# Scatter behind the first level, folds dealt evenly, and experts walked in their own order

## The reference

```python
# 1. delta-rule attention; B, H, S, D = 4, 8, 768, 48
k_n = k / (norm(k) + 1e-6)
for t in range(S):
    y[t] = q[t] @ state
    state = state + beta[t] * outer(k_n[t], v[t] - k_n[t] @ state)
x = y as (3072 tokens, 384)
# 2. dense part, d_model 384, d_ff 1024
h = (x @ w1) * (x @ w2) @ w3
x = h @ w_out
# 3. 8 experts, one for each token
logits = x @ w_gate + modality_bias[modality_id]
e_idx = argmax(logits);  gate_w = softmax(logits)[e_idx]
out[token] = gate_w * (relu(x @ moe2_w1[e_idx]) @ moe2_w2[e_idx])
```

## Time and profile before

| what | value |
|---|---|
| runs | 986.44, 989.28, 988.99 us; median 988.99 us |
| profiled execution | 982.71 us, its span 980.8 us |
| PE busy | 889.7 us (91%) |
| DVE, ACT, POOL busy | 497.3, 343.7, 277.7 us |
| DMA | 60.13 MB, mean 61 GB/s |
| mean granted clock of TensorE | 0.955 |
| last dense product ends, about | 678 us |
| first down products of the expert stage | 727.4 us |

### The profile page before, as it was taken

The page is one execution under the profiler, slowest core; times in us unless marked ns, Lnnn a source line. Parts: engine busy times, 40 slices in busy tenths (PEclk is TensorE's granted clock), DMA queues, the critical chain, the costliest instruction groups (busy, mean ns, idle before and its releaser), DMA issues.

```text
span 980.8 us, 29550 instructions
## 1 busy us (share of the span) xinstructions
PE 889.7 (91%) x11972; PEld 746.7 (76%) x11973; DVE 497.3 (51%) x891; ACT 343.7 (35%) x628; POOL 277.7 (28%) x296
## 2 busy tenths in 40 slices
PE   4898878999998999899989999997369999999996
PEld 3666556778876887688768878986259898989985
DVE  2456656665675567556755673232356333333332
ACT  1234343443554355435533442221153222222221
POOL 5333333444434443444344421010001101011010
PEclk9999986999999999999989999998579999999998
DMA  7333211111111111111111101100941111111110
GB/s 248 104 103 113 75 37 37 38 38 38 47 39 58 38 44 42 59 38 46 40 59 30 29 23 46 32 34 18 320 181 44 42 42 41 38 41 41 48 42 21
DMA packets 46570, 60.13 MB, mean 61 GB/s; under 512 B 9192, under 2 KB 39160, under 8 KB 45552
## 3 DMA queue, kind: packets, MB, share of 16 engines
q1 hardware_dynamic: 38640, 42.35, 14.4%
q0 software_dynamic: 3200, 9.56, 2.6%
q10 hardware_dynamic: 4608, 6.46, 2.5%
HBM read 42.26 MB, written 11.77 MB: 55 GB/s over the span
## 4 chain that ended last, share of the span: by engine, by line
PE 76%; POOL 7%; DVE 6%; issue 5%; ACT 3%; DMA 1%; SPq 1%; ACTq 0%; POOLq 0%; DVEq 0%
PE banks L1418 17%; PE banks L1543 12%; PE banks L1557 11%; PE banks L1436 10%; PE banks L1278 4%; PE banks L1388 3%; PE banks L1355 2%; PE banks L1574 2%; PE banks L1345 2%; PE banks L1367 2%; PE banks L1238 2%; POOL nm L535 1%; POOL inv L539 1%; DVE corr L873 1%; POOL sorted_rows L555 1%
## 5 line engine op out<-in xcount | busy, mean ns | idle before, releaser
L1418 PE MATMUL banks<-xr,w12r 128*128 128x512 f32 x864 | 226.4, 410 | 0.0
L1418 PEld LDWEIGHTS banks<-xr,w12r 128*128 128x128 f32 x864 | 159.9, 193 | 35.9 <-DVE xr L933 0.2
L1543 PE MATMUL banks<-experts,kept 128*128 x486 | 124.6, 411 | 11.0 <-DVE experts L1170 8.5
L1543 PEld LDWEIGHTS banks<-experts,kept 128*128 128x128 f32 x486 | 92.6, 195 | 32.3 <-issue 11.6
L1557 PE MATMUL banks<-experts,kept 128*128 x624 | 114.8, 340 | 0.0
L1436 PE MATMUL banks<-kept,hr 128*128 128x392 f32 x576 | 112.2, 347 | 0.0
L1557 PEld LDWEIGHTS banks<-experts,kept 128*128 128x128 f32 x624 | 107.1, 188 | 0.0
L1436 PEld LDWEIGHTS banks<-kept,hr 128*128 128x128 f32 x576 | 100.9, 188 | 2.0
L585 POOL DMA_INDIRECT out<-ys,xs x26 | 25.6, 984 | 259.8 <-DVE ys L1205 259.8
L523 POOL TENSOR_TENSOR kb<-keys,beta_sb 128x384 f32<-128x384 f32 x24 | 29.1, 1214 | 245.5 <-PE banks L1377 245.5
L621 ACT ACTIVATE inv<-banks 128x512 f16<-128x512 f32 x96 | 57.2, 596 | 84.9 <-PE banks L1278 72.4
(11 more groups left out here) (144 smaller groups left out, 1338.9 us busy)
## 6 DMA issues: line engine op xcount, KB each, us to landing
raw<-in_moe_w SPq DMA_DIRECT2D x6, 1536.0 KB, 7.3
kq<-in_qT SPq DMA_DIRECT2D x24, 256.0 KB, 2.7
xs<-sorted_rows ACTq DMA_DIRECT2D x28, 197.0 KB, 2.4
kraw<-in_k SPq DMA_DIRECT2D x24, 192.0 KB, 2.3
vals<-in_v SPq DMA_DIRECT2D x48, 96.0 KB, 2.5
w3T<-in_w3T SPq DMA_DIRECT2D x8, 512.0 KB, 4.4
w<-in_w SPq DMA_DIRECT2D x8, 384.0 KB, 4.7
xT<-yT SPq DMA_DIRECT2D x48, 64.0 KB, 2.1
```

What stands on the lines that cost most here:

```text
L1418: last = mm(psum[:, UP + w, :], w12r[:, p, w, k, j * P:(j + 1) * P], xr[:, r, k, :], start=(k == 0 and p == r), stop=(k == KT - 1 and p == 1))
L1543: last = mm(psum[:, f, :], xsr[:, w, p, k, :], experts[:, bass.ds(slot * (2 * WE) + at, FF // 2)], start=(k == 0 and p == r), stop=(k == K ...
```

## The change

Four parts.

- **Scatter.** POOL's `scatter` of turn u moves to turn u+1, behind `first_level` and ahead of `square`.
- **Gates and folds.** The 24 gate products of turn 0 are dealt four to each of the six slots. The 64 fold products are dealt evenly over the 30 slots of turns 1 to 5. Copies and loads follow the block that ends.
- **Experts in their own order.** The table's expert is the expert's number; the tile count of an expert is at least one; SP loads experts 0 to 7 without conditions. Ten operations on VectorE that made ranks are gone.
- **Early loads and splits.** `xs` and `raw` change places in memory. SP loads experts 0 and 1 when attention has ended; ScalarE and VectorE split expert 0 at pieces 17, 20 and 21 of the last group; expert 1 is split by ScalarE behind the last `exps` (w1) and behind the first two tiles' rows (w2), by VectorE behind these rows (w1) and the first hidden values (w2). `table[3]` starts at 1, so tile 0 splits nothing.

```diff
@@ -35,6 +35,7 @@
 PIECES = 24
 FIRST_GROUP = 6
 FIRST_SLOT = 2
+FOLD_SLOTS = SPLITS * (FIRST_GROUP - 1)
 E_SCALE = 1024.0
 ROW = WX + 2
 GATE, TOKEN = WX, WX + 1
@@ -48,6 +49,7 @@
 NO_TOKEN = 1 << 20
 
 ROWS = (18, 19, 22, 23)
+FIRST_SPLITS = {17: ("w1", 0), 20: ("w1", 1), 21: ("w2", 0)}
 CHOOSE, EXPS, COUNT, WEIGH, RANK = 2, 3, 4, 6, 9
 
 
@@ -184,8 +186,8 @@
         late = ExitStack()
         experts = sbuf(late, "experts", [P, SLOTS * 2 * WE], F32R)
         hid = sbuf(late, "hid", [P, FF])
+        xs = sbuf(late, "xs", [P, TURN, ROW])
         raw = sbuf(late, "raw", [P, SLOTS * WE])
...
         def gates_of(u, at):
 
-            return range(8 * (at // 2), 8 * (at // 2) + 8) if u == 0 and at % 2 else range(0)
+            return range(4 * at, 4 * at + 4) if u == 0 else range(0)
 
         def folds_of(u, at):
 
-            half = (0, None, 1, 2, None, 3)[at] if at != 1 and at != 4 else None
-            if half is None or not 1 <= u <= 4:
-                return []
-            i = 2 * (u - 1) + half // 2
-            return [(i, half % 2)]
+            n = SPLITS * (u - 1) + at
+            return range(FT * FT * n // FOLD_SLOTS, FT * FT * (n + 1) // FOLD_SLOTS) if 0 <= n < FOLD_SLOTS else range(0)
+
+        def folds_ended(u, at):
+
+            return [n // FT for n in folds_of(u, at) if n % FT == FT - 1]
+
+        def fold_turn(i):
+
+            return next(u for u in range(1, FIRST_GROUP) for at in range(SPLITS) if i in folds_ended(u, at))
 
         def piece_of(u, at):
...
                     load_k(u + 3)
-                for n in (2 * u - 1, 2 * u):
-                    if W_SLOTS <= n < FT:
+                for n in range(W_SLOTS, FT):
+                    if u == fold_turn(n - W_SLOTS) + 1:
                         load_w3(n)
+                    if n in (2 * u - 1, 2 * u):
                         load_w12(n)
                 if live(u) and u:
                     load_v(u)
...
                 sp.wait_ge(sent[b], 64 * C)
             sp.wait_ge(q["y_taken"], UNITS + 1)
+            def load_expert(k):
+
+                for at, size, name in ((0, KT * FF, "w1"), (KT * FF, FT * DM, "w2")):
+                    since(sp, q[f"expert_{name}_in"], 16 * k)
+                    if k >= SLOTS:
+                        sp.wait_ge(q[f"lower_{name}"], (k - SLOTS + 1) * (2 if name == "w1" else 1))
+                    at_slot = k % SLOTS * WE + at
+                    sp.dma_start(raw[:, at_slot:at_slot + size], a[f"moe2_{name}"][k]
+                                 ).then_inc(q[f"expert_{name}_in"], 16)
+
             sp.dma_start(fill[:], a["fill"]).then_inc(q["b_in"], 16)
             sp.dma_start(numbers[:], a["small"][:, M_STARTS:]).then_inc(q["b_in"], 16)
 
 
+            for k in range(SLOTS):
+                load_expert(k)
             sp.wait_ge(q["b_in"], 80)
             sp.dma_start(sorted_rows[E * CAP:E * CAP + P, :], fill[:, :].bitcast(F32)
                          ).then_inc(q["filled"], 16)
 
             fill_after(sp, range(0, E, 2))
 
-            sp.wait_ge(q["ranks_ready"], 1)
-            for k in range(E):
-                e = sp.value_load(table[0:1, 2, k:k + 1], min_val=0, max_val=E - 1)
-                some = sp.value_load(table[0:1, 2, E + k:E + k + 1], min_val=0, max_val=1)
-                with sp.If(some > 0):
-                    at_slot = k % SLOTS * WE
-                    for at, size, name in ((0, KT * FF, "w1"), (KT * FF, FT * DM, "w2")):
-                        if k == 0 and name == "w2":
-
-                            for w in range(2):
-                                sp.wait_ge(x_in[w], 16)
-                        if k:
-
-                            sp.wait_ge(q[f"expert_{name}_in"], 16 * k)
-                        if k >= SLOTS:
-
-                            sp.wait_ge(q[f"lower_{name}"], (k - SLOTS + 1) * (2 if name == "w1" else 1))
-                        sp.dma_start(raw[:, at_slot + at:at_slot + at + size],
-                                     a[f"moe2_{name}"][bass.ds(e, 1)].rearrange("o p n -> p (o n)")
-                                     ).then_inc(q[f"expert_{name}_in"], 16)
+            for k in range(SLOTS, E):
+                load_expert(k)
 
 
         @block.gpsimd
...
             def turn(u):
                 if live(u):
                     first_level(u)
+                for at in range(SPLITS):
+                    piece = piece_of(u - 1, at)
+                    if piece and piece[0] and piece[1] == RANK:
+                        scatter(piece[0] - 1)
                 if live(u + 2):
                     square(u + 2)
                 if live(u + 1):
@@ -566,10 +582,6 @@
                     beta_keys(u + 1)
                 if live(u + 2):
                     normalise(u + 2)
-                for at in range(SPLITS):
-                    piece = piece_of(u, at)
-                    if piece and piece[0] and piece[1] == RANK:
-                        scatter(piece[0] - 1)
 
             nc.gpsimd.memset(keys[:, :, D:PAD], 0.0).then_inc(q["key_pad_clear"], 1)
...
                 for c in group_begun(u, at, 2):
                     split_x(c)
+
+            def upper_ahead(rank, name, f=0):
+                act.wait_ge(q["up_b"], FT * C)
+                if rank:
+                    act.wait_ge(q["down_done"], B * C)
+                act.wait_ge(q[f"expert_{name}_in"], 16 * (rank + 1))
+                src, upper, _ = ahead_of(rank, name, f)
+                nc.scalar.activation(upper, src, ACT.Copy).then_inc(q[f"upper_{name}"], 1)
 
             def turn(u):
                 if live(u - 1):
@@ -766,6 +787,8 @@
             for u in range(-2, last_turn() + 1):
                 turn(u)
             exps(C - 1)
+            upper_ahead(1, "w1", 0)
+            upper_ahead(1, "w1", 1)
 
 
...
@@ -800,13 +823,10 @@
             act.wait_ge(q["filled"], 16 * (E + 1))
             load_x(0, 0)
             load_x(1, 1)
-            first = act.value_load(table[0:1, 3, 0:1], min_val=0, max_val=E - 1)
-            split(first, "w1", [0])
             take_x(0, 0)
-            split(first, "w1", [1])
             take_x(1, 1)
+            upper_ahead(1, "w2")
             take_hid(0)
-            split(first, "w2")
 
...
@@ -1029,12 +1049,16 @@
 
                 v.tensor_copy(place[:], lred[:, 4]).then_inc(q["place_ready"], 1)
 
+            def lower_ahead(rank, name, f=0):
+                dve.wait_ge(q[f"upper_{name}"], 2 * rank + f + 1 if name == "w1" else rank + 1)
+                src, upper, lower = ahead_of(rank, name, f)
+                nc.vector.tensor_tensor(lower, src, upper, ALU.subtract).then_inc(q[f"lower_{name}"], 1)
+
...
@@ -1113,45 +1139,32 @@
             v.tensor_tensor(fill_at[:], small[:, M_PLACE:M_PLACE + E], total, ALU.add
                             ).then_inc(q["fill_ready"], 1)
             link(v.tensor_reduce(ntile[:, 0], over[:], AX.X, ALU.add))
-            link(v.tensor_scalar(ntile[:, 1], ntile[:, 0], 0.0, None, ALU.is_gt))
-
-            link(v.tensor_copy(ntile[:, 2:4, 0:1], ntile[:, 0:2, 0:1]))
+            link(v.tensor_scalar(ntile[:, 0], ntile[:, 0], 1.0, None, ALU.max))
+
+            link(v.tensor_copy(ntile[:, 1, 0:1], ntile[:, 0, 0:1]))
             for e in range(1, E):
-                link(v.tensor_tensor(ntile[:, 2:4, e:e + 1], ntile[:, 2:4, e - 1:e], ntile[:, 0:2, e:e + 1],
-                                     ALU.add))
+                link(v.tensor_tensor(ntile[:, 1, e:e + 1], ntile[:, 1, e - 1:e], ntile[:, 0, e:e + 1], ALU.add))
             tiles = numbers[:, M_TILE - M_STARTS:M_TILE - M_STARTS + TABLE * E].rearrange("p (i e) -> p i e", e=E)
 
-            def by_tile(k, n=TABLE):
-                return ntile[:, None, k, :].to_broadcast([P, n, E])
-
-
-            link(v.tensor_tensor(past[:, 0, 0:E], tiles[:, 0:E], by_tile(3, E), ALU.is_ge))
-            link(v.tensor_reduce(ttab[:, 0, 0:E], past[:, 0, 0:E], AX.X, ALU.add))
-            v.tensor_scalar(table[:, 2, 0:E], ttab[:, 0, 0:E], float(E - 1), None, ALU.min)
-            link(v.tensor_scalar(ttab[:, 2, 0:E], numbers[:, M_TILE - M_STARTS:M_TILE - M_STARTS + E * E:E],
-                                 ntile[:, 3, E - 1:E], None, ALU.is_lt))
-            v.tensor_copy(table[:, 2, E:2 * E], ttab[:, 2, 0:E]).then_inc(q["ranks_ready"], 1)
-            v.tensor_copy(table[:, 2, 2 * E:2 * E + 1], ntile[:, 2, E - 1:E])
-
-
-            link(v.tensor_tensor(past[:, 0], tiles, by_tile(2), ALU.is_ge))
+            def by_tile(k):
+                return ntile[:, None, k, :].to_broadcast([P, TABLE, E])
+
+            v.tensor_copy(table[:, 2, 2 * E:2 * E + 1], ntile[:, 1, E - 1:E])
+
+
+            link(v.tensor_tensor(past[:, 0], tiles, by_tile(1), ALU.is_ge))
             link(v.tensor_tensor(past[:, 1], past[:, 0], by_tile(0), ALU.mult))
             link(v.tensor_reduce(ttab[:, 0], past[:, 0], AX.X, ALU.add))
             link(v.tensor_reduce(ttab[:, 1], past[:, 1], AX.X, ALU.add))
```

(31 more changed lines are left out.)

29 lines of the change are left out of this document (19 added, 10 removed).

## The result

**Slower, as forecast, by a little more.** The changed kernel takes 1054.94 us (median of 4 runs, 1054.72 to 1055.84), the kernel before 987.72 (4 runs, 986.05 to 989.28): ratio 1.0683, 95% interval 1.0659 to 1.0706. Forecast were 1049 us and a range of 1028 to 1075. The profiled execution took 1054.83 us, its span is 1053.0 us. In the frame of profiled executions, where the sum was made, 1042.3 stood against 1054.8: the sum was 12.5 us short, and half of that was made up in the total by the 6.3 us added for the median. The kernel after doesn't show such a difference (its median and its profiled execution agree).

A forecast was written before the change was run, and what follows sets the result against it. TensorE bounds the expert stage, a chain of small products and copies the attention turns. 982.7 + 87 (stalled tiles) - 12.4 (early loads) - 15 (folds) + 0 (scatter) = 1042.3; plus 6.3 for the median: 1049 us, range 1028 to 1075.

The forecast's parts named there:

- 6.3 us added for the median: Whole kernel: the median of the runs lies 6.3 us above the profiled execution, taking 1042.3 to 1049.
- 31 tiles, 16 transfers, five stalls: Expert stage: five empty experts add tiles, 26 to 31; tiles with a split just begun stall, 87 us in all.
- 17.4 us a stalled tile: One-tile experts: split ready at +6.5, then 8.8, plus 2.1 for the clock; bounds 15.3 and 24.1.
- Rivals 1 (no stall): Expert stage: splits keep ahead, so extra tiles cost 48 us instead of 87; total 1010, chance 6%.
- 2 (low clock throughout, 24.1): Expert stage: TensorE at the low level all through one-tile experts, 34 us more; total 1082, chance 9%.
- rival 4: Expert stage: an empty expert takes no tile after all, leaving only -12.4 and -15; total 962, chance 3%.
- Smaller folds and gates, -15: Attention turns 0 to 6: evenly dealt products shorten gaps on the chain, -15 us; bounds -21 and -5.
- Rival 3: Attention turns 0 to 5: smaller folds give nothing because TensorE's waits keep the clock low; total 1064, chance 9%.
- Early loads and splits, -12.4: Change of stage: experts 0 and 1 prepared early bring tile 1's transposes from 731.64 to 719.2, -12.4 us.
- Extra ahead of the fills and the x loads: 0: Change of stage: expert 2's transfers, issued earlier by SP, delay nothing, 0 us; one transfer more would cost 4.9.
- Scatter behind the first level, 0: Three scatter turns: the wait only moves from `turn_first` to `sums`, 0 us; bounds -3 and +1.6 a turn.
- the term for the clock: Scatter turns: a low-clock stretch on the chain from the longer single wait, taken at 0, bound +1.6 us a turn.

The follow-up runs named there:

- after_kept_busy: The kernel after with 22 unread products on TensorE ahead of the waiting up products of the first three stalled tiles; 1049.73 us, ratio 1.0641.
- experts_alone: The kernel after with scatter and gate and fold products as in the kernel before; 1063.34 us, ratio 1.0763.
- folds_alone: The kernel before with only the new dealing of gate and fold products and their w3 loads; 973.31 us, ratio 0.9857.

## Why the prediction was right, point by point

- **31 tiles, 16 transfers, five stalls.** Right, and read from counts alone: three of eight experts used, `max(.., 1)`, and the expert of tile 1 split ahead.
- **17.4 us a stalled tile.** Measured 17.2. All its parts, read from a tile of before in which nothing waited, came out: the split ready at +6.5 (so again), 8.8 behind it (after_kept_busy: periods of 15.3 to 15.6, the 15.3 of the sum), and 2.1 for the clock, measured 1.7 to 1.9. Here rule and trace were weighed. The rows: products behind a wait of 5.44 us take 6.39 us, behind a gap of 0.28 us 4.47. The Trainium skill (TensorE: Matmul & The Clock Gate, Part 1, What's actually happening) has the throttled state as the default that activity lifts; by that rule, the trace agrees. Rivals 1 (no stall) and 2 (low clock throughout, 24.1) fall, and with the 31 tiles rival 4.
- **Smaller folds and gates, -15.** Measured -12.7 in the kernel after and -13.5 alone. Turns 1 to 3 last 20.9, 20.6 and 20.5 us as forecast, turn 0 gives 3.2 of 3.3. What is missing lies in turns 4 (0.6 won) and 5: the "about 1.5" for turn 5 isn't there (22.6 us against 22.2), where the last fold waited 2.02 us, to 127.86, for its w3, whose load was issued at 122.67: the bound that the prediction named. Rival 3 falls.
- **Early loads and splits, -12.4.** Measured -9.5. The step that failed is "Extra ahead of the fills and the x loads: 0", argued from one transfer that stood beside them before also. With both transfers of expert 2 ahead, the rows landed in 6.66 us instead of 3.45. The prediction held the price of one transfer, 4.9, as its bound, and 3.2 of that was due. The Trainium skill (DMA: Bandwidth & Descriptors, Issuing engines are not separate DMA queues) says that transfers of all issuers interleave on the same engines. The trace agrees, with 43 packets of one queue beside 186 of the other; how much a small transfer loses by it, that section doesn't say.
- **Scatter behind the first level, 0.** Measured +4.7 over three turns. The move of the wait from `turn_first` to `sums` was right, its length nearly so ("some 5.5", measured 6.00 on VectorE and 4.64 on TensorE), and so was "its result comes when it came before": the second pair starts 15.9, 15.7 and 15.7 us into the three turns, against 15.8, 15.7 and 16.4. The step that failed is the term for the clock, taken at 0 with +1.6 a turn as its bound: the products behind the single longer wait ran at the low level, on the chain. All of the loss arises between the second and the third pair: 2.4, 1.6 and 0.7 us, so the bound covers two of the three turns.
- **Turn 24, in no step.** Between the two traces 4.5 us lie here, with a "remote" wait of 6.8 us on ScalarE. It is no consequence of the change, as experts_alone and folds_alone show, but of which execution of before was traced.

```profile
584.81 0.60 ACT L639 ACTIVATE inv<-banks 128x512 f16<-128x512 f32 x1 [6.83 <-remote]
```

- **The remainder.** 2.3 (folds) + 4.7 (scatter) + 4.5 (turn 24) + 2.9 (x rows) - 1.1 (stalls) = 13.3 us: the difference between 72.9 and 59.6 at the last tile. Without the 4.5, 8.8 us are the prediction's own misses. The total came within 6 us with the help of the 6.3 added for the median, for which the prediction had no cause. The stop of turn 24, which the traced execution of before lacks, may be most of it; that isn't shown, and as far as the prediction goes it was luck.
